# The order of ScalarE's work in the steps of an mLSTM and slot-expert kernel: transfers last, one copy ahead of the gates, and the logits of two chunks first

## Time and profile before

| | before |
|---|---|
| median of 3 runs | 386.51 us (386.49 to 386.62) |
| the profiled execution's own time | 386.7 us |
| its span, from first to last instruction | 385.0 us |
| PE busy | 366.2 us (95%) |
| PEld busy | 309.5 us (80%) |
| DVE busy | 236.1 us (61%) |
| ACT busy | 230.3 us (60%) |
| POOL busy | 81.7 us (21%) |
| mean granted clock of TensorE | 1.000 of full speed |

### The profile page before, as it was taken

The page is one execution under the profiler, slowest core; times in us unless marked ns, Lnnn a source line. Parts: engine busy times, 40 slices in busy tenths (PEclk is TensorE's granted clock), DMA queues, the critical chain, the costliest instruction groups (busy, mean ns, idle before and its releaser), DMA issues.

```text
span 385.0 us, 9592 instructions
## 1 busy us (share of the span) xinstructions
PE 366.2 (95%) x3506; PEld 309.5 (80%) x3506; DVE 236.1 (61%) x557; ACT 230.3 (60%) x459; POOL 81.7 (21%) x122
## 2 busy tenths in 40 slices
PE   2999999989998999999999999999999999999996
PEld 2687767767676866435599999999999999999996
DVE  8767568558845864620787565565565556556553
ACT  3467668567665854221587576666666656667662
POOL 7276557346644641000000000000000000000000
PEclk9999999999999999999999999999999999999999
DMA  6489798797788696989500010010001001001001
GB/s 182 109 255 302 244 256 270 209 246 245 238 218 270 211 308 196 363 281 328 202 0 3 0 70 0 2 68 0 0 17 51 0 0 68 0 0 70 2 0 68
DMA packets 28024, 51.49 MB, mean 134 GB/s; under 512 B 2868, under 2 KB 19700, under 8 KB 27732
## 3 DMA queue, kind: packets, MB, share of 16 engines
q1 hardware_dynamic: 25028, 40.49, 34.5%
q10 hardware_dynamic: 2960, 10.51, 8.5%
HBM read 46.59 MB, written 4.33 MB: 132 GB/s over the span
## 4 chain that ended last, share of the span: by engine, by line
PE 88%; DVE 4%; ACT 4%; issue 2%; ACTq 1%; DMA 1%; POOL 0%; DVEq 0%
PE heads_banks L1169 7%; PE high_banks L1171 7%; PE high_banks L1170 7%; PE high_banks L1169 7%; PE heads_banks L1170 7%; PE heads_banks L1171 7%; PE low_banks L1151 6%; PE heads_banks L853 6%; PE low_banks L832 5%; PE heads_banks L846 3%; PE high_banks L868 3%; PE low_banks L812 3%; PE low_banks L885 3%; PE low_banks L1075 2%; PE low_banks L903 2%; PE high_banks L876 2%
## 5 line engine op out<-in xcount | busy, mean ns | idle before, releaser
L752 ACT ACTIVATE relu_h<-low_banks 128x512 f32<-128x512 f32 x95 | 56.9, 599 | 60.0 <-PE low_banks L1151 59.6
L1492 DVE CAST sq_hi<-sq_h 128x512 fp32r<-128x512 f32 x95 | 40.6, 427 | 65.5 <-ACT sq_h L757 65.0
L1494 DVE TENSOR_TENSOR sq_lo<-sq_h,sq_hi 128x512 fp32r<-128x512 f32 x95 | 65.8, 692 | 3.3
L757 ACT ACTIVATE sq_h<-relu_h 128x512 f32<-128x512 f32 x95 | 60.0, 632 | 3.0
L1169 PE MATMUL heads_banks<-wo_hi,sq_hi 128*128 128x320 f32 x192 | 59.2, 308 | 0.6 <-DVE sq_lo L1494 0.4
L1171 PE MATMUL high_banks<-wo_hi,sq_lo 128*128 128x320 f32 x192 | 59.4, 309 | 0.0
L1170 PE MATMUL high_banks<-wo_lo,sq_hi 128*128 128x320 f32 x192 | 59.4, 309 | 0.0
L1169 PE MATMUL high_banks<-wo_hi,sq_hi 128*128 128x320 f32 x192 | 59.4, 309 | 0.0
L1171 PE MATMUL heads_banks<-wo_hi,sq_lo 128*128 128x320 f32 x192 | 59.3, 309 | 0.0
L1170 PE MATMUL heads_banks<-wo_lo,sq_hi 128*128 128x320 f32 x192 | 59.2, 308 | 0.0
L1211 DVE TENSOR_TENSOR att_w<-low_banks,att_w 128x512 f32<-128x512 f32 x48 | 30.9, 685 | 32.3 <-PE low_banks L832 31.6
(11 more groups left out here) (190 smaller groups left out, 551.3 us busy)
## 6 DMA issues: line engine op xcount, KB each, us to landing
w_sb<-in_w SPq DMA_DIRECT2D x8, 1280.0 KB, 11.7
w_a<-in_w ACTq DMA_DIRECT2D x16, 512.0 KB, 5.6
kv_in<-in_kv SPq DMA_DIRECT2D x24, 320.0 KB, 4.2
qk_in<-in_qk SPq DMA_DIRECT2D x24, 256.0 KB, 3.6
o_in<-in_o_gate SPq DMA_DIRECT2D x24, 160.0 KB, 4.0
out<-out_sb SPq DMA_DIRECT2D x5, 640.0 KB, 3.2
wo_raw<-in_w_out SPq DMA_DIRECT2D x4, 640.0 KB, 12.9
w_b<-in_w ACTq DMA_DIRECT2D x8, 256.0 KB, 4.8
```

The source lines that it names most:

```text
L752: act.activation(relu_h[:, slot], bank[slot][:, :], ACT.Relu).then_inc(relu_done, 1)
L757: act.activation(sq_h[:, slot], relu_h[:, slot], ACT.Square).then_inc(sq_done, 1)
L1492: dve.tensor_copy(sq_hi[:, slot], sq_h[:, slot]).then_inc(hi_done, 1)
L1494: dve.tensor_tensor(sq_lo[:, slot], sq_h[:, slot], sq_hi[:, slot].bitcast(F32), ALU.subtract).then_inc(lo_done, 1)
```

## The change

Three edits. In `load_w1` the eight `w1_b` transfers are issued one at a time, in the steps n with n mod 5 equal to 3 or 0 up to 20 (in those with 3, a `w1_a` is issued too), and `load_w1` is called at the end of ScalarE's step and not between the fade and the gates. The copy of the second half of the combine weights is made ahead of the gates in the last step of a batch; that of the first half stays where it was. In `logit`, the products of the first two chunks of the triple over the two 128-row parts are issued first, behind a wait for those two chunks only; then comes the wait for the third chunk and the rest. In the very last triple, whose first two chunks and third chunk are already separate calls, the order stays.

```diff
@@ -618,10 +618,10 @@
                 if n % 5 > 0 and n - n // 5 <= len(W1_PARTS):
                     e, k = W1_PARTS[n - n // 5 - 1]
                     act.dma_start(w1_a[:, e, k], w1[e, P * k:P * (k + 1), :]).then_inc(w1_loaded, 16)
-                if n > 0 and n % 5 == 0:
-                    for e in range(2 * (n // 5 - 1), 2 * (n // 5)):
-                        p0 = DP * (e // 4)
-                        act.dma_start(w1_b[p0:p0 + DM_LAST, e % 4], w1[e, 2 * P:DM, :]).then_inc(w1_loaded, 16)
+                if n % 5 in (0, 3) and 0 < n <= 20:
+                    e = 2 * (n // 5) - (n % 5 == 0)
+                    p0 = DP * (e // 4)
+                    act.dma_start(w1_b[p0:p0 + DM_LAST, e % 4], w1[e, 2 * P:DM, :]).then_inc(w1_loaded, 16)
 
             def dispatch_exp(rb):
 
@@ -684,12 +684,14 @@
                     copy_heads(b, c)
                     if c < NC - 1:
                         raise_fade(b, c + 1)
-                    load_w1(step(b, c))
+                if rb is not None and c == NC - 1:
+                    copy_comb(rb, 1)
+                if cur:
                     half_tanh(b, c)
                 if prev:
                     copy_xT(*before(b, c))
-                if rb is not None and c >= 4:
-                    copy_comb(rb, c - 4)
+                if rb is not None and c == NC - 2:
+                    copy_comb(rb, 0)
                 if rb is not None and c == 1:
                     dispatch_exp(rb)
                 if prev and before(b, c)[1] % TRI == TRI - 1:
@@ -698,6 +700,8 @@
                     weigh_thirds()
                 if rb is not None and c == 1:
                     row_exps(rb)
+                if cur:
+                    load_w1(step(b, c))
 
             for c in range(NC):
                 act_step(0, c, 0, prev=c > 0)
@@ -893,14 +897,18 @@
 
             def logit(b, c, thirds=range(TRI)):
 
-                pe.wait_ge(xT_ready, step(b, c) - 1 + thirds[-1])
                 pe.wait_ge(phi_loaded, 32)
                 if b < B - 1 or c < NC - 1:
                     pe.wait_ge(fade_ready, rescales(*after(*after(b, c))))
-                for k in range(KC):
+                ahead = [(k, q) for k in range(KC - 1) for q in thirds if q < TRI - 1]
+                rest = [(k, q) for k in range(KC) for q in thirds if (k, q) not in ahead]
+                if ahead:
+                    pe.wait_ge(xT_ready, step(b, c))
+                for n, (k, q) in enumerate(ahead + rest):
                     rows = slice(0, min(P, DM - P * k))
-                    for q in thirds:
-                        mm = pe.matmul(logit_ps[QUAD * q:QUAD * (q + 1), :], phi_sb[rows, k], xT[rows, k, q], start=k == 0, stop=k == KC - 1)
+                    if n == len(ahead):
+                        pe.wait_ge(xT_ready, step(b, c) - 1 + thirds[-1])
+                    mm = pe.matmul(logit_ps[QUAD * q:QUAD * (q + 1), :], phi_sb[rows, k], xT[rows, k, q], start=k == 0, stop=k == KC - 1)
                 if TRI - 1 in thirds:
                     mm.then_inc(logits, 1)
 
```

## The result

The changed kernel takes 384.04 us, the median of five runs (383.95 to 384.88). The kernel before, run beside it, takes 386.62 us (five runs, 386.49 to 387.37). The ratio is 0.9931 with an interval of 0.9916 to 0.9946: faster by 2.67 us, between 2.1 and 3.25. The forecast was 384.4 us, a gain of 2.05. The sign and the mechanism held.

What follows compares the result with a forecast made beforehand. TensorE was taken to bound the kernel, with 88% of the span. Gains of 2.70 less costs of 0.65 gave net 2.05 us, so 386.51 would become 384.45, said as 384.4, range 383.7 to 385.5.

Steps and rivals of the forecast that it cites:

- The combT wait: State matmuls after a batch's last step stop waiting for the combine-weight copy: 0.68 us gained twice, 1.36 in all.
- The cover: After the earlier state matmuls, decay matmuls would come at 83.03, behind the xT copy ending at 82.59: 0.4 us spare.
- The transfers: Stalls from paired w1_b issues go: gains 0.66 at (0,5), 0.31 at (1,4), 0.32 at (2,3), 0.05 at (3,2).
- The last step: In (3,5) the combine copy delays gates, xT and everything behind: 0.37 us lost, bounds 0 and 0.4.
- The issues in the new place: Transfers issued before the next step's decays fit or are covered: cost 0, bounds 0 and 0.7 us.
- rival 3: One issue runs long once in a step issuing two transfers: 0.7 us lost, time 385.1, chance 0.09.
- The logits: Issuing two chunks' products first costs 0.04 us at each of seven sites, 0.28 in all; bounds -0.05 and 0.7.
- rival 1: Strict order in the logits, third strip behind passes ahead: seven sites lose 0.10 each, time 384.9, chance 0.17.

Runs made afterwards that it cites:

- experiment 2: Kernel before with only the second combine-weight copy moved ahead of the gates in a batch's last step: 386.13 us, ratio 0.9972.
- Experiment 3: Kernel before with all w1 transfers issued at the end of ScalarE's step, w1_b still in pairs: 385.72 us, ratio 0.9965.
- experiment 4: Kernel before with the w1_b transfers spread over eight steps but issued in the old place, between fade and gates: 385.97 us, ratio 0.9972.
- experiment 1: Kernel before with the logits edit alone, two ready chunks' products issued first: 386.62 us, ratio 0.9991.
- experiment 5: Kernel after with the second combine copy put behind the xT copy in the last step (3,5) only: 383.89 us, again 383.74 us.
- Experiment 8: Kernel after with four transfers, one w1_a and three w1_b, issued at the end of step (2,1): 384.55 us, ratio 0.9941.
- Experiment 7: Kernel before with only the order of waits changed, xT listed first before the seven logits groups, nothing issued ahead: 386.61 us, ratio 0.9992.
- experiment 6: Kernel after with one logits product issued ahead of the third chunk's wait instead of four: 384.37 us, ratio 0.9932.
- experiment 10: Kernel after with the last step's combine copy behind xT, and xT's wait listed first before last logits and decay matmuls: 383.67 us, ratio 0.9916.

## Why the prediction was right, and where it wasn't

- **The combT wait, 1.36.** Right: 1.37 in the trace, and by itself (experiment 2) the same. The cover held, the copy of xT still waits 0.61 for TensorE.
- **The transfers, 0.66 + 0.31 + 0.32 + 0.05.** Right: 1.41 in the trace; only (3,2), at 0.12, lies above its bounds of 0 and 0.1. Experiment 3 shows that their place alone does it, and experiment 4 that spreading alone gives nearly as much with a part paid elsewhere. One thing the prediction did not know: the pair that gave the 0.66 was long by chance, in three of four traces. With a short pair the trace of experiment 1 lost that wait without any edit, so the lasting worth of this term lies between 0 and 0.66, by how often the pair is long. That the forecast took its 0.66 from a single execution and met it is in part luck. That experiment 3 gained 1.35 us by its ratio too suggests that the pair was long in most executions.
- **The last step, -0.37.** Right: 0.38, taken back whole by experiment 5.
- **The issues in the new place, cost 0.** Right. The issues ran long in double steps (those with a `w_a` and a `w_b`) more often than rival 3 had it: `w_b` took 1.37 in (1,2) and 1.10 in (2,1), and 1.50 in (2,1) of a later run, which cost 0.1 there in passing and nothing elsewhere. The prediction let the issues begin behind the last work of the step. They began sooner: in (2,1) the `w_a` issue starts at 91.98, while `disp_e`, which stands before it in the program, starts at 92.17. So ScalarE's issues don't keep the strict order that the section on the kernel before gives every engine. Experiment 8 shows where the cover ends, at 0.64 us of late decays.
- **The logits, +0.28: the failed step.** "It can't gain more than 0.01. I take 0.04 a site, 0.28 in all." It was -0.06 a site, and with +0.05 and +0.09 at the two short groups -0.28 in all. This is 0.56 of the 0.66 us by which the trace's sum (2.71) exceeds the prediction's (2.05). The mistake is in the words "as soon as its data is there, at 87.94": 87.94 was the start of the matmuls, and the data was there at 87.84, when the copy ended. The "0.19 <- issue" in the earlier trace rows was read as the ordinary state of an engine with nothing to wait for, and a quarter of it (0.047) was the cost of a wait in the wrong place. Experiment 7 put it in order without touching anything else. That the passes drawn ahead cost and gain next to nothing by themselves, as the prediction had it, was right (experiment 6). Also the third strip does not stand behind the passes drawn ahead. In the trace of the kernel after, at the site in (2,0), its first pass is the one whose weight load carries the wait for xT. It starts at 86.015, 0.052 after the copy's end (85.963), and four passes of the two strips ahead of it in program order start after it, between 86.045 and 86.160. The other six sites show the same to a few nanoseconds. Behind its first, each strip's own passes are 0.11 apart. So strict order (rival 1) isn't what this array does with three strips of 32 columns. The Trainium skill, TensorE: Matmul & The Clock Gate, section "The mechanism", says that matmuls start and end strictly in program order; for the starts this trace doesn't agree.

The forecast of 384.4 came within 0.4 of the measured time because this term was small. Had the logits edit been the whole change, the forecast would have had the wrong sign.

Left open: what prolongs single issues (in the kernel before, one of SyncE's own took 1.85 us at the moment of the long pair, but in experiments 2 and 7 the pair was as long and SyncE's issue beside it took 0.45 and 0.37); how often the first pair is long; and the place of the `w_out` split.

## What to carry to other kernels

When the bound engine waits for another, ask of every instruction between the wanted result and its producer what it is worth there: 0.68 us a time came from one copy moved ahead of work that waits anyway, and in the one step that had no such slack the same move cost 0.38. Put transfer issues in front of an instruction that waits for someone else, and work out how late that one may be. And where a matmul shows idle time under "issue" behind a signal that has just come, look at the order of its waits: list the one that comes last first. It is worth 0.05 to 0.12 us a time here, too little for the timings to confirm.

## What the runs showed of the hardware

- The wait listed first is carried by the weight load, and the matmul starts 0.05 us after the signal. A signal that is waited for behind it costs more: listing it first gave 0.047 us a time at the logits (experiment 7), 0.09 at the last logits and 0.12 at the decay matmuls (experiment 10).
- fp32 passes in different 32-column strips of the array start out of program order (86.015 against 86.045 to 86.160); passes of one strip come 0.11 us apart, 0.13 behind the first.
- One `w_b` issue of the same shape takes 0.47 to 0.72 us on ScalarE in 96 of the 112 cases in the fourteen traces, and 1.0 to 1.5 in fifteen. All issues of `w_b` in the kernel after (line, issuing engine, KB each not listed, ns min/median/max, first and last):

```profile
L624 ACTq DMA_DIRECT2D w_b<-in_w x8: 473/511/1366, 39.2 to 130.5; - x8
```

- The first decay matmuls start anywhere from 15.9 to 16.5 us in different executions. A difference of 0.5 us between two single profiles can be just that.
